# Attention in thirds with sinks a tile ahead, and k and q stored so that a third is one DMA

## What is computed

```python
scores = scale * (q @ k.T)                    # B=2, H=8, S=768, D=64
keep = (pos_k < 4) | ((rel >= 0) & (rel < 128))
a = softmax(where(keep, scores, -1e9));  x = a @ v
x = x.transpose(0, 2, 1, 3).reshape(1536, 512)
out = x where x @ w_skip <= 0, else x + gate * relu(x @ w1[e]) @ w2[e]
h = out @ w_in;  g = P(h) / Q(h);  result = g @ w_out
```

## Time and profile before

| | us |
|---|---|
| median of three runs | 630.32 |
| profiled execution, its own time | 631.54 |
| its span, first to last instruction | 629.8 |
| attention, first load issued to last x_tok | 2.25 to 167.5 |
| mean granted TensorE clock over the span | 0.945 |

### The profile page before, as it was taken

How to read it: one execution, slowest core, us unless ns; L and a number is a source line. 1 busy time by engine, 2 the same in 40 slices (tenths; PEclk the granted TensorE clock), 3 DMA queues, 4 the chain that set the end, 5 groups by cost and what they waited for, 6 DMA issues and landing times. The chain is left out here.

```text
span 629.8 us, 9524 instructions
## 1 busy us (share of the span) xinstructions
PE 562.7 (89%) x3152; PEld 486.4 (77%) x3153; DVE 440.3 (70%) x471; ACT 306.8 (49%) x615; POOL 320.7 (51%) x245
## 2 busy tenths in 40 slices
PE   5669788799886999999978869999999999999996
PEld 5558777688786899999967648888888888888884
DVE  2699897987145142654442899999888888888883
ACT  2554545456350133443423646766656555765553
POOL 3444352420002265445502958779886667666673
PEclk9597978899998799999998979999999999999999
DMA  8781909930294385999903112110200000100001
GB/s 164 159 180 43 209 1 186 376 106 0 92 390 170 90 329 203 340 399 399 361 33 117 52 52 66 50 51 17 97 22 18 1 1 1 67 1 0 1 0 67
DMA packets 37780, 77.31 MB, mean 123 GB/s; under 512 B 3120, under 2 KB 14384, under 8 KB 37744
## 3 DMA queue, kind: packets, MB, share of 16 engines
q1 hardware_dynamic: 33616, 64.79, 33.3%
q0 software_dynamic: 2832, 9.70, 4.8%
q10 hardware_dynamic: 1296, 2.36, 1.0%
HBM read 63.21 MB, written 13.63 MB: 122 GB/s over the span
## 5 line engine op out<-in xcount | busy, mean ns | idle before, releaser
L1363 DVE RECIPROCAL den<-den 128x512 f32<-128x512 f32 x48 | 160.8, 3350 | 30.6 <-POOL den L1154 30.6
L1217 PE MATMUL moe_h_ps<-x_hi,work 128*128 128x512 f32 x384 | 99.2, 401 | 8.4 <-DVE g L1368 8.2
L1154 POOL TENSOR_TENSOR den<-den,side 128x512 f32<-128x512 f32 x48 | 62.2, 1297 | 65.8 <-ACT den L1290 65.7
L1217 PEld LDWEIGHTS moe_h_ps<-x_hi,work 128*128 128x128 f32 x384 | 72.9, 191 | 26.7 <-DVE g L1368 9.0
L1236 PE MATMUL o_ps<-w_out_hi,g_hi 128*128 128x512 f32 x192 | 76.5, 399 | 0.4 <-ACT g_hi L1312 0.4
L1237 PE MATMUL o_ps<-w_out_lo,g_hi 128*128 128x512 f32 x192 | 75.8, 395 | 0.0
L863 PEld LDWEIGHTS h_ps<-xT,w_sb 128*128 128x128 f32 x576 | 68.4, 199 | 2.3 <-issue 1.7
L863 PE MATMUL h_ps<-xT,w_sb 128*128 128x128 f32 x576 | 68.7, 282 | 1.4 <-ACT xT L890 1.4
L1147 POOL TENSOR_TENSOR g_lo<-g,g_hi 128x512 fp32r<-128x512 f32 x48 | 63.1, 1315 | 11.0 <-ACT g_hi L1312 11.0
L1156 POOL TENSOR_TENSOR g<-g,square 128x512 f32<-128x512 f32 x48 | 63.5, 1324 | 1.7 <-ACT g L1295 1.7
L311 PE MATMUL out_ps<-v_sb,probsT 128*128 128x128 f32 x352 | 53.7, 314 | 6.0 <-DVE x_tok L411 6.0
(11 more groups left out here) (168 smaller groups left out, 1063.9 us busy)
## 6 DMA issues: line engine op xcount, KB each, us to landing
w_raw<-in_w SPq DMA_DIRECT2D x32, 512.0 KB, 6.4
w_sb<-in_w SPq DMA_DIRECT2D x8, 2048.0 KB, 11.2
k_raw<-in_k SPq DMA_DIRECT2D x16, 384.0 KB, 7.2
q_raw<-in_q SPq DMA_DIRECT2D x16, 384.0 KB, 9.6
rows_dram<-zero_rows SPq DMA_DIRECT2D x1, 4864.0 KB, 18.2
w_in_raw<-in_w_in POOLq DMA_DIRECT2D x8, 512.0 KB, 5.6
w_out_raw<-in_w_out SPq DMA_DIRECT2D x16, 256.0 KB, 2.6
v_sb<-in_v SPq DMA_DIRECT2D x4, 768.0 KB
```

The lines of the kernel that those rows point to most:

```text
L1154: pool.tensor_tensor(den[d][:], den[d][:], side[c % 2][:], ALU.add).then_inc(den_ready, 1)
L1217: mm = pe.matmul(h_ps[bank % HB][:], w[:, k, f], x[:, k, :], start=n == 0 and k == 0, stop=n == len(parts) - 1 and k == z.KD - 1)
L1363: nc.vector.reciprocal(den[d][:], den[d][:]).then_inc(inv_ready, 1)
```

## The change

The host stores q and k by batch entry, half of the heads and third of the sequence: for each third 64 rows of 4 x 256 numbers, 4 KB together. A third of a group is loaded with one DMA; its source is the 64 rows with a leading step of 0 and count 2, its destination all 128 partitions. Loads, casts and subtractions go by thirds, and each third has its own semaphores. The loops over b are unrolled.

Sinks are scored a tile ahead in each slot, with keys scaled and gathered in `k_sink`; VectorE sums them from PSUM straight into `probs`. The negation is done in the maximum. v gets two more columns a head, the first of them ones, so that the products with v hold the row sums too; v is loaded head by head in runs of 256 bytes (four DMAs a group instead of one). `evacuate_sinks` and the casts of q go to ScalarE, VectorE keeps those of k. GpSimd's first instructions are in another order and there are four more selects for the ones beside the sinks. TensorE waits for the identity alone before its warm-up, and does a few products more in four slots (`FILL`).

```diff
-    STEPS = 2 * z.QT
-    LAG_T, LAG_O, LAG_N = 2, 3, 4
-    LAG_H = 3
-    HALVES = ((0, z.S // 2), (z.S // 2, z.S))
+    GROUPS = 2 * z.B
+    STEPS = GROUPS * z.QT
+    LAG_T, LAG_O = 2, 3
+    THIRDS = z.THIRDS
+    THIRD = z.S // THIRDS
     WARM_UP = 24
-    SINK_STEPS = 2 * (z.QT - 2)
+    FILL = {2: 8, 3: 4, STEPS + 1: 4, STEPS + 2: 8}
+    SINK_TILES = z.QT - 2
...
-        raw = [sb(f"{n}_raw", [P, G, z.S]) for n in "kq"]
-
+        raw = [sb(f"{n}_raw", [P, THIRDS, G, THIRD]) for n in "kq"]
...
-            with sp.Fori(0, z.B) as b:
-                for g in range(2):
-
-                    sp.wait_ge(split_ready[1 - g], 1 + 2 * (b + g))
-                    heads = slice(g * G, (g + 1) * G)
-                    for n, (lo, hi) in enumerate(HALVES):
-                        for src, dst, loaded in zip((k, q), raw, raw_loaded[n]):
-                            for part in (slice(0, z.DH), slice(z.DH, P)):
-                                sp.dma_start(dst[part, :, lo:hi], src[bass.ds(b, 1), heads, :, lo:hi].rearrange("o h d s -> d (o h) s")).then_inc(loaded, 16)
-
-                    sp.wait_ge(zeroed, 6)
-
-                    sp.wait_ge(v_used[g], 1 + b)
-                    src = v[bass.ds(b, 1), :, g * GC:(g + 1) * GC].rearrange("o (i p) c -> p (o i) c", p=P)
-                    sp.dma_start(v_sb[g][:, :, 0:GC], src).then_inc(v_loaded[g], 16)
-                    for h in range(G):
-                        c = g * GC + h * z.DH
-                        sp.dma_start(v_sink[g][h * n_sink:(h + 1) * n_sink, h * z.DH:(h + 1) * z.DH],
-                                     v[bass.ds(b, 1), 0:n_sink, c:c + z.DH].rearrange("o n c -> (o n) c")).then_inc(v_loaded[g], 16)
+            for n in range(GROUPS):
+                b, g = n // 2, n % 2
+                heads = slice(g * G, (g + 1) * G)
+                for p in range(THIRDS):
+                    count, c = n * THIRDS + p, third(p)
+                    if n > 0:
+
+                        sp.wait_ge(k_low_ready, count - THIRDS + 1)
+                    sp.dma_start(raw[0][:, p].rearrange("p h s -> p (h s)"), k[b, g, p].unsqueeze(0).to_broadcast([2, z.DH, G * THIRD])).then_inc(k_loaded[p], 16)
+                    if n > 0:
+
+                        sp.wait_ge(q_low_ready, count - THIRDS + 1)
+                    sp.dma_start(raw[1][:, p].rearrange("p h s -> p (h s)"), q[b, g, p].unsqueeze(0).to_broadcast([2, z.DH, G * THIRD])).then_inc(q_loaded[p], 16)
+
+                if n == 0:
+                    sp.wait_ge(zeroed, 8)
+                    sp.wait_ge(sink_ones, 4)
+                if n >= 2:
+
+                    sp.wait_ge(normed, (n - 1) * z.QT)
+                for h in range(G):
+                    c = g * GC + h * z.DH
+                    sp.dma_start(v_sb[g][:, :, h, 0:z.DH], v[b, :, c:c + z.DH].rearrange("(i p) c -> p i c", p=P)).then_inc(v_loaded[g], 16)
+                    sp.dma_start(v_sink[g][h * n_sink:(h + 1) * n_sink, h, 0:z.DH], v[b, 0:n_sink, c:c + z.DH]).then_inc(v_loaded[g], 16)
...
+            for count in range(1, GROUPS * THIRDS):
+                n, p = divmod(count, THIRDS)
+                g, c = n % 2, third(p)
+                q_hi = q_split[g][z.DH:, :, c]
+
+                pool.wait_ge(k_high_ready, count + 1)
+                pool.wait_ge(k_low_ready, count)
+                pool.wait_ge(q_low_ready, count)
+                pool.tensor_tensor(k_split[g][:, 1, :, c], raw[0][:, p], k_split[g][:, 0, :, c].bitcast(F32), ALU.subtract).then_inc(k_low_ready, 1)
+
+                pool.wait_ge(q_high_ready, count + 1)
+                pool.wait_ge(k_low_ready, count + 1)
+                pool.tensor_tensor(q_hi, raw[1][z.DH:, p], q_hi.bitcast(F32), ALU.subtract).then_inc(q_low_ready, 1)
...
+            def fill(j):
+
+                if j in FILL:
+
+                    pe.wait_ge(masked, min(j - 1, STEPS))
+                    keep_warm(pe, keep, scores_ps[j % 2][:, 0, 0:P], FILL[j])
...
+                if 1 <= i < z.QT - 1:
+
+                    if i == 1:
+                        pe.wait_ge(k_sink_ready, n + 1)
+                    if i % 2 == 1:
+                        pe.wait_ge(q_low_ready, n * THIRDS + (i + 1) // 2 + 1)
+                    if sink_step(j + 1) > 0:
+
+                        pe.wait_ge(sinks_placed, sink_step(j + 1))
+                    if j >= 4:
+
+                        pe.wait_ge(normed, j - 3)
+                    for h in range(G):
+                        mm = pe.matmul(sink_scores_ps[:, h], q_of(g, h, i + 1), k_sink[g][:, h], start=True, stop=True)
                     mm.then_inc(sinks_scored, 1)
...
-            def weigh(b, j):
-                e, g, i = place(b, j)
+            def weigh(j):
+                n, i = place(j)
+                b, g = n // 2, n % 2
                 if i == 0:
-                    pe.wait_ge(v_loaded[g], 16 * (1 + G) * (e + 1))
-                pe.wait_ge(evacuated, 2 * done(b, j))
-
-                pe.wait_ge(normed, done(b, j - 1))
+                    pe.wait_ge(v_loaded[g], 32 * G * (b + 1))
+                if j >= 1:
+
+                    pe.wait_ge(normed, j)
                 if i >= 2:
-                    pe.wait_ge(sink_evac, (e + 1) * SINK_STEPS + g * (z.QT - 2) + i - 1)
-
-                    pe.matmul(out_ps[:, :, 0:z.DH], sink_probsT[j % 2][:], v_sink[g][:].rearrange("p (h d) -> p h d", h=G),
-                                   start=True, stop=False, skip_group_check=True)
-
-
+                    pe.wait_ge(sink_evac, sink_step(j) + 1)
+
+                    pe.matmul(sums_ps, sink_probsT[j % 2][:], v_sink[g][:], start=True, stop=False, skip_group_check=True)
                 for h in range(G):
-                    c = slice(h * z.DH, h * z.DH + P)
+                    if h % 2 == 0:
+                        pe.wait_ge(evacuated, 2 * j + h // 2 + 1)
                     for side in range(1 if i == 0 else 0, 2):
-                        mm = pe.matmul(out_ps[:, h, :], probsT[j % 2][:, h, side, :], v_sb[g][:, i - 1 + side, c],
+                        mm = pe.matmul(sums_ps[:, h, :], probsT[j % 2][:, h, side, :], v_sb[g][:, i - 1 + side, h, :],
                                        start=i < 2 and side == (1 if i == 0 else 0), stop=side == 1, skip_group_check=True)
                 mm.then_inc(summed, 1)
...
+            def high_k_act(p):
+
+                act.wait_ge(k_loaded[p], 16)
+                act.activation(k_split[0][:, 0, :, third(p)], raw[0][:, p], ACT.Copy).then_inc(k_high_ready, 1)
+
+            def high_q(count):
+
+                n, p = divmod(count, THIRDS)
+                act.wait_ge(q_loaded[p], (n + 1) * 16)
+                if count > 0:
+                    act.wait_ge(q_high_ready, count)
+                act.activation(q_split[n % 2][:, :, third(p)], raw[1][:, p], ACT.Copy).then_inc(q_high_ready, 1)
+
+            def sink_keys(n):
+
+                g = n % 2
+                act.wait_ge(k_low_ready, n * THIRDS + 1)
...
+                act.activation(k_sink[g][:], k_split[g][:, :, :, 0:n_sink].rearrange("p w h n -> p h w n").bitcast(F32),
+                               ACT.Copy, scale=SCALE).then_inc(k_sink_ready, 1)
+
...
+                if i >= 2:
+                    act.activation(sink_probsT[j % 2][:], sink_probsT_ps, ACT.Copy).then_inc(sink_evac, 1)
+
+            def exponentials(j):
+                n, i = place(j)
                 lo, hi = cols(i)
-                act.wait_ge(negated, done(b, j))
-
-                act.wait_ge(normed, done(b, j - LAG_N))
+                act.wait_ge(negated, j + 1)
                 for h in range(G):
                     row = probs[j % 2][:, h, lo:hi]
-                    act.activation(row, row, ACT.Exp, bias=neg_max[j % 2][:, h:h + 1], scale=1.0,
-                                   accum_out=row_sum[j % LAG_N][:, h:h + 1]).then_inc(exped, 1)
+                    act.activation(row, row, ACT.Exp, bias=neg_max[j % 2][:, h:h + 1], scale=1.0).then_inc(exped, 1)
                 if i >= 2:
 
-                    act.wait_ge(exped, G * done(b, j))
-                    act.wait_ge(transposed, 2 * done(b, j - 2))
+                    act.wait_ge(exped, G * (j + 1))
+                    if j >= 2:
+                        act.wait_ge(transposed, 2 * (j - 1))
                     act.activation(sink_probs[j % 2][:].rearrange("p (h n) -> p h n", h=G), probs[j % 2][:, :, 2 * P:W], ACT.Copy).then_inc(sinks_packed, 1)
 
-            walk(act, [(LAG_T, evacuate), (1, exponentials)])
+            high_k_act(0)
+            high_k_act(1)
+            high_q(1)
+            sink_keys(0)
+            for j in range(STEPS + LAG_T):
+                if 0 <= j - LAG_T < STEPS:
+                    evacuate(j - LAG_T)
+                if 0 <= j - 1 < STEPS:
+                    exponentials(j - 1)
+                    n, i = place(j - 1)
+                    if j == 1:
+                        high_k_act(2)
+                        high_q(2)
+                    if n + 1 < GROUPS:
```

(125 more changed lines are left out.)

224 lines of the change are left out of this document (83 added, 141 removed).

## The result

766.64 us median of 4 runs (763.22 to 767.62), against 630.56 (629.43 to 631.87) for the kernel before on the same chip: ratio 1.2137, 95% interval 1.2082 to 1.2193. The kernel became a fifth slower. The profiled execution took 766.97 us, its span 765.3.

A forecast was written before the change was run, and what follows sets the result against it. Bound before: VectorE standing behind GpSimd. After: 24 two-engine loads take 245.8 us, last q lands at 262.7, attention ends at 300.5 against 167.5, 133 us more, giving 764 us; range 585 to 795.

The forecast's parts named there:

- (g): Loads of q and k: each third runs on two DMA engines, 10.24 us; 24 of them take 245.8 us.
- SP issues 6 instead of 8 a group and they cost it nothing: SP's load issues: one DMA a third means fewer issues a group, at no cost to SP.
- (a) to (f): Edits inside the attention step: VectorE gets back 35.7 us of 152; TensorE is next late, compute some 117 us.
- rival B: Loads of q and k run on all 16 engines and stay hidden; attention ends at 128, kernel 591 to 606; chance 0.27.
- VectorE standing behind GpSimd as the old bound: Attention before: small VectorE instructions wait out GpSimd's 3.47 us subtraction; such steps are 7.13 us apart, others 4.16.
- (a): Scaled sink copy L384 goes, sum taken from PSUM into probs: 22.6 us at 16 instructions becomes 4.6.
- (b): Negation L391 moves into the reduction: 13.4 us of VectorE goes.
- (d): row_sum becomes a column of ones in v, read from PSUM; VectorE's count unchanged, normalising one slot late.
- The extra keep-warm products lie in idle slots and cost nothing: TensorE's added products (8, 4, 4, 8) cost nothing in idle slots, under 1 us in a busy one.
- Rival C: All engines, but normalising waits for the products in a closed loop: slots 7.2 us instead of 6.3, kernel 646; chance 0.03.
- Rival D: Two engines per transfer but others each time: 10 us latency in front, hidden later; 600 us; chance 0.04.

The follow-up runs named there:

- e13_no_stalls_right: Kernel before with q and k rows stored twice, negation fused into the maximum, sinks scaled once a group and placed by a reduction, row_den a reduction; 598.83 us.
- e12_no_stalls: Kernel before with q and k rows stored twice, negation fused into the maximum, sinks placed by a sum and left unscaled; 621.62 us.
- e2: The changed kernel with each q and k row stored twice in HBM, so both DMA sides have 128 rows; 590.37 us, ratio 0.9343.

## Why the prediction was right

764 us forecast, 766.6 measured. By its own steps:

- **(g), two engines for every load**: right, 10.2 us a load at 52 GB/s, shown with counts 2, 4, 8 and 128. The last q was to land at 262.7; its cast starts at 264.2. That this is so close is partly luck. The first load was issued at 0.81 instead of 2.25 us, and 24 loads at the measured 10.17 us make 244.1 instead of 245.8; against that v and the gaps between groups took 16.5 us (264.2 less 0.8, 2.8 of overhead and 244.1) where I had 12. Behind the last q the clock was priced well: from its cast to the exponentials of tile 23 it took 26.9 us, forecast 27.8 with 4 for the clock, and the granted clock was 0.57 from 264 to 280 us. The end came 11.6 us after these exponentials began, instead of the 10.0 that I took from the old order. Attention ended at 302.6 for 300.5.
- **"SP issues 6 instead of 8 a group and they cost it nothing"**: wrong. SP stands up to 17 us in an issue of k or q, and the next group's first load is late by it. It is a part of the 4.5 us by which v and the gaps exceed their 12; how large a part wasn't separated.
- **(a) to (f) and the new bound**, tested in rival B: attention at 126.7 for 128, the kernel at 590.4 for 591, a group every 26.2 us (softmax of the first tile of three groups at 36.78, 63.13 and 89.19) for 26. L384 is now 0.19 us 16 times, 3.0 us for the 4.6 forecast, and TensorE is the next late. The first score came at 9.67 us, forecast 10.7. The sum of rival B has 114 us from four groups and the tail and goes on with 117, 3 us that no row of it gives; the measured 117.0 (126.7 less 9.67) is luck to that extent.
- **VectorE standing behind GpSimd as the old bound**: right, `e13_no_stalls_right` takes 29.8 us off the old attention by that alone. But what (a) and (b) do gave 20.0 of these in `e12_no_stalls`: row_den took over 13.6 us of the standing. In the rebuilt order (d), which was said to leave VectorE's count alone, also keeps row_den out of it, since it reads PSUM.
- **"The extra keep-warm products lie in idle slots and cost nothing"**: wrong in the part, 2.3 us on the path at the start; in the sum no cost or gain can be told from the spread. In the changed kernel itself the start doesn't count, since the loads set the end.
- **Rival C** (the closed loop) didn't come: before the tail e2's row_den waits for out_ps only three times, 1.2 us each at the first tile of a group; the last three tiles wait 10.0 of the 13.4 us in all. **Rival D** (other pairs each time) is out: within a group the loads land 10.2 to 11.5 us apart, at some 50 GB/s.

## What to carry to other kernels

Read both sides of a DMA: an outer count under 16 on either side limits how many engines run (shown here for 2, 4 and 8 in the source). A broadcast source of two copies makes a wide, well-shaped transfer a two-engine one; store the rows twice (590.4 us) or issue a DMA a half (597.7 us). Where a small VectorE instruction on SBUF alone has a mean many times its unstalled duration, look in the timeline whether it ends together with an instruction of GpSimd. Removing one such instruction can move the wait to the next, as it did to row_den, so replace all of them (reductions, or operands in PSUM) before judging.
